# Moving the first tile's residual add and its low parts ahead of the sums in DVE's queue

## The reference

```
q_d, k_d, v_d = means over groups of 4 positions
out_d     = softmax(q_d k_d^T / 8) v_d               # 144 positions
out_up    = repeat(out_d, 4)                         # back to 576
out_local = softmax(q k^T / 8 where |i-j| < 4) v     # banded
x = out_up + out_local                               # tokens x 512
h = x @ w_in;  x = (h * tanh(softplus(h))) @ w_out   # d_ff 2048
h = x @ w_in2; s = h * softmax(h)                    # d_ff 1024
x = layernorm(s) * g_ln @ w_out2
```

## Time and profile before

| | |
|---|---|
| median of 3 runs | 734.22 us (733.68 to 735.09) |
| the profiled execution | 736.92 us, its span 735.1 us |
| PE busy | 703.1 us, 96% |
| DVE, ACT, POOL busy | 333.2, 244.1, 93.2 us |
| mean granted clock of PE | 0.981 |

### The profile page before, as it was taken

One profiled execution on the slowest core, in us unless ns is written; L12 is line 12 of the kernel. 1 busy time (PEld: TensorE's weight loads), 2 busy tenths in 40 slices (PEclk: granted clock), 3 DMA queues, 4 the chain that ended last, 5 costly groups with the idle time before them and its releaser, 6 DMA issues.

```text
span 735.1 us, 12338 instructions
## 1 busy us (share of the span) xinstructions
PE 703.1 (96%) x5152; PEld 646.4 (88%) x5152; DVE 333.2 (45%) x640; ACT 244.1 (33%) x525; POOL 93.2 (13%) x123
## 2 busy tenths in 40 slices
PE   6778779999999999999999999999999999999997
PEld 5667668999999999999999999999788888888886
DVE  7996986553222223322232332124854444445441
ACT  5676676332211211121121112115543333343432
POOL 5785760000000000000000000002000000000000
PEclk9897899999999999999999999999999999999999
DMA  8996765000000000000000000005000000000001
GB/s 227 209 264 174 224 215 217 1 1 1 1 1 0 1 1 1 1 1 0 1 1 1 1 0 1 1 1 228 1 28 17 29 15 30 15 29 15 29 15 44
DMA packets 24423, 37.50 MB, mean 51 GB/s; under 512 B 2480, under 2 KB 12720, under 8 KB 24368
## 3 DMA queue, kind: packets, MB, share of 16 engines
q1 hardware_dynamic: 24368, 36.71, 16.5%
HBM read 31.99 MB, written 4.72 MB: 50 GB/s over the span
## 4 chain that ended last, share of the span: by engine, by line
PE 81%; DVE 10%; issue 4%; ACT 3%; DMA 1%; POOL 1%; SPq 0%; POOLq 0%; DVEq 0%; ACTq 0%
PE psum L537 27%; PE psum L551 25%; PE psum L631 12%; PE psum L607 11%; PE psum L617 2%; DVE xy L930 1%; DVE xy L939 1%; DVE prob L905 1%; ACT prob L701 1%; DVE mx L902 1%; PE psum L523 1%; PE psum L508 1%; DVE wlo L1020 1%; DMA kT<-kT_dram 1%; DVE den L912 1%
## 5 line engine op out<-in xcount | busy, mean ns | idle before, releaser
L983 DVE CAST ghi<-g_sb 128x384 fp32r<-128x384 f32 x96 | 34.5, 360 | 260.9 <-PE psum L551 204.0
L725 ACT ACTIVATE g_sb<-psum 128x384 f32<-128x384 f32 x96 | 47.2, 492 | 302.8 <-PE psum L537 302.8
L537 PE MATMUL psum<-xhi,whi 128*128 128x384 f32 x384 | 129.8, 338 | 0.6 <-DVE wlo L949 0.4
L537 PE MATMUL psum<-xlo,whi 128*128 128x384 f32 x384 | 129.3, 337 | 0.0
L537 PE MATMUL psum<-xhi,wlo 128*128 128x384 f32 x384 | 129.2, 336 | 0.0
L551 PE MATMUL psum<-ghi,wlo 128*128 128x384 f32 x384 | 129.0, 336 | 0.0
L551 PE MATMUL psum<-ghi,whi 128*128 128x384 f32 x384 | 129.0, 336 | 0.0
L551 PE MATMUL psum<-glo,whi 128*128 128x384 f32 x384 | 129.0, 336 | 0.0
L537 PEld LDWEIGHTS psum<-xhi,whi 128*128 128x128 f32 x384 | 72.4, 189 | 1.4 <-ACT g_sb L725 0.7
L537 PEld LDWEIGHTS psum<-xlo,whi 128*128 128x128 f32 x384 | 72.5, 189 | 0.0
L537 PEld LDWEIGHTS psum<-xhi,wlo 128*128 128x128 f32 x384 | 72.4, 189 | 0.0
(11 more groups left out here) (95 smaller groups left out, 938.3 us busy)
## 6 DMA issues: line engine op xcount, KB each, us to landing
wraw<-w_dram SPq DMA_DIRECT2D x16, 512.0 KB, 7.1
qT<-qT_dram SPq DMA_DIRECT2D x16, 288.0 KB, 4.1
kT<-kT_dram SPq DMA_DIRECT2D x16, 288.0 KB, 6.0
v<-v_dram SPq DMA_DIRECT2D x16, 288.0 KB
out_dram<-ob SPq DMA_DIRECT2D x18, 256.0 KB, 2.0
vw<-v_dram SPq DMA_DIRECT2D x32, 128.0 KB, 4.0
wraw<-w_dram SPq DMA_DIRECT2D x4, 1024.0 KB, 7.0
vw<-v_dram SPq DMA_DIRECT2D x32, 32.0 KB, 4.0
```

The lines of the kernel that those rows point to most:

```text
L537: ins = nc.tensor.matmul(bank, a[:, w], b[:, kdx, :], start=(kdx == 0 and n == 0), stop=(kdx == KD - 1 and n == 2))
L725: nc.scalar.activation(g_sb[:, f % HR, :], psum[:, HB1 + f % HB, 0:N1], ACT.Mish).then_inc(g_ok, 1)
L983: nc.vector.tensor_copy(ghi[:, f % GR, :], g_sb[:, f % HR, :]).then_inc(ghi_ok, 1)
```

## The change

In each DVE turn the add and the low part now stand between `maxima_pooled(u)` and `sum_local(u)`, while ACT exponentiates the local scores, and no longer last in the turn. The low part of chunk 3 stays where it was, in turn 16 (it is not in the new place, since that is only reached for u < 16, and the line in turn 16 is unchanged).

```
                 if u < UNITS:
                     subtract_local(u)
                     maxima_pooled(u)
+
+                    if u in ADDED:
+                        add_pooled(0, ADDED.index(u))
+                    if u - 1 in ADDED:
+                        split_x(0, ADDED.index(u - 1))
                     sum_local(u)
...
                 if u >= LATE:
                     evict_local(u - LATE, 1)
-
-                if u in ADDED:
-                    add_pooled(0, ADDED.index(u))
-                if u - 1 in ADDED[:KD - 1]:
-                    split_x(0, ADDED.index(u - 1))
                 if u == UNITS - 1:
                     weights_in_low(0)
```

## The result

The changed kernel takes 727.7 us in the median of four runs (723.8 to 729.0), the kernel before 734.65 us; the ratio is 0.9892, 95% interval 0.9845 to 0.9939. Six more runs of it, beside 17 of the kernel before on the same chip, gave 728.2 us (726.8 to 729.4) and a ratio of 0.9911, interval 0.9887 to 0.9936. So it is faster by about 1%, 6 to 7 us. I had forecast 722.8 us, 11.4 less. By its median the first measurement lies 0.2 us beyond the upper end of my range; by its ratio, set against the 734.22 us from which I had worked, it is 726.3 us and inside. Of 11.4 us some 7 came, and what is missing needs an explanation.

A forecast was written before the change was run, and what follows sets the result against it. Attention turns: three engines nearly full, DVE most, and the add held up by POOL stops three engines. Savings 3.45 + 2.5 + 3.41 + 2.0 = 11.4 us, off the 734.2 us median: 722.8 us, range 717.0 to 727.5.

The forecast's parts named there:

- The add in its new place: Turns 3, 7, 11: the add gets POOL's pause behind pbias, takes about 0.6 us, turn 5.2 us.
- the pause on which I had set 1.7 us: Turn 7, POOL between half_qk and qd, 0.08 us long: an add missing it costs 1.7 us more.
- rival (b)'s second half: Adds of turns 7 and 11 miss POOL's pause: 2 x 1.7 us more, 726.2 us; whole rival 0.23.
- ACT's wait: ACT waited 14.4 us in four waits for the add before copying xhi; wait and following low clock would go.
- One short add stops three engines: Attention turns: a 2.52 us add left ACT idle 4.15 us and TensorE without work 4.16 us, then at 1.2 GHz.
- The low part: Turns 4, 8, 12: it waits 1.1 us for half_v and works 0.5, adding 1.5 us; turn 6.4 us.
- rival (c): Moved instructions get in between any two of POOL's; low parts cost some 0.5 us, 719.8 us; chance 0.06.
- only where POOL pauses for its own semaphore: A DVE add with two SBUF inputs gets in only at such POOL pauses, delaying POOL's next by 0.2 us.
- I keep one such pause: Turns 7 to 9: one TensorE pause costing about 5.2 us stays, so 2.5 us is saved, not 7.69.
- (a): No TensorE pause at all, instructions come in time: 16.6 us saved, 717.6 us; chance 0.20.
- (b): Losses return: second late load or instruction page, 728.0 us, or adds missing POOL's pause, 726.2; chance 0.23.
- The end: Up to the first expert product: it starts 1.4 us sooner, with 0.6 us of clock loss back, together 2.0.

The follow-up runs named there:

- adds_only: Changed kernel with only the adds moved, the low parts staying last in their turn: 725.8 us, ratio 0.9888.
- after_split: Changed kernel with the first weights' piece 0 issued in halves in SP's steps 13 and 16, piece 1 in step 17: 721.6 us, ratio 0.9833.
- after_no_v8: Changed kernel without 14 of the 16 loads of v for pooling: 720.4 us, ratio 0.9821.
- before_late: Kernel before with the two 1 MB pieces of the first weights issued in SP's steps 13 and 15, not 8 and 13: 735.0 us, ratio 1.0011.
- before_no_v8: Kernel before without 14 of the 16 loads of v for pooling: 733.9 us, ratio 0.9979.
- the early pieces: Changed kernel with both 1 MB pieces of the first weights issued in SP's steps 7 and 8: 727.55 us.

## Why the prediction was right, and where it was not

**The add in its new place** was right: 0.69, 0.69 and 0.55 us in turns 3, 7 and 11, POOL's next instruction later by 0.2 to 0.3 us, den's slack taking up most of it. In turn 7 it missed the pause on which I had set 1.7 us; it got in one instruction later, in front of kd, so that rival (b)'s second half would have been worth nothing:

```profile
43.76 0.43 POOL L402 TENSOR_TENSOR qd<-half_qk 128x144 f32<-128x144 f32 x1
...
43.91 0.69 DVE L939 TENSOR_TENSOR xy<-xy,od 128x384 f32<-128x384 f32 x1
...
44.14 0.74 POOL L402 TENSOR_TENSOR kd<-half_qk 128x144 f32<-128x144 f32 x1
```

**ACT's wait** went, and the low clock with it in turns 4 and 12 (in turns 8 and 9 the pauses kept it low, 0.77 and 0.56). As the reason of the gain it was overrated: ACT a turn later gives back 0.95 us of turns 3 and 4, the moved add 3.0 (adds_only), add and low part together 4.1. "One short add stops three engines" was true, but the engine whose stop set the length was DVE. The sum did not suffer, since I had worked it out from turns as a whole.

**The low part** was mis-sized: 1.5 us each, measured 0.72, 0.55 and 0.73 (the 0.55 in turn 8, where POOL stood waiting for v). That is rival (c), which I gave 0.06, and the rule of the Trainium skill (SBUF — State Buffer, "SBUF: two separate sides") that stands beside it: whichever instruction starts first has the ports. I had taken the place of half_v from turn 6 of the kernel before, where it began 0.03 us before pbias; behind an add POOL is later, and qd was still running. The trace of after_split, with half_v first in turn 8, has the 1.60 us, that of after_no_v8 1.46. My reading "only where POOL pauses for its own semaphore" is refuted, and the Trainium skill's rule isn't enough either: it doesn't give the 2.52 us of the old place or the 1.41 us above.

**What was left out: POOL.** I had noted that three engines are nearly full and then gave turns 5 and 6 the old 4.67 and 4.91 us. With the gaps gone, POOL has no time to catch up: turns 5, 6, 13 and 14 took 5.01, 5.44, 5.01 and 5.30 us, 1.8 us more than before in all (their sum in the kernel before is 18.98). That eats most of what the low parts saved, and adds_only shows both sides of it: with the low part in its old place turn 4 takes 6.62 us and not 5.50, but turns 5 and 6 take 4.67 and 5.10.

**The step that failed** is "I keep one such pause". First, the pause of 2.56 us was in the profiled execution of the kernel before and, as before_late and before_no_v8 suggest, mostly not in its median; I took a saving read from a span of 735.1 us off a median that lay 2.7 us below its execution. Secondly, after the change there were three in the profiled execution, and they cost 7 to 8 us: 728.2 with all loads, 720.4 without those of v. I had set down the saturation as the case against (a) and for (b), and gave (b) 0.23; its 728.0 us came nearest. The figure that I had for it was weak, though: 205 to 226 GB/s is not what a full queue moves at most, for the earlier trace rows have 282 and 306 GB/s at shares of 1.09 and 0.95, and the changed kernel moved 223 to 262 in turns 3 to 6 without a pause over 1.1 us. Without pauses on either side my terms give 3.45 + 3.36 + 3.41 + 2.0 = 12.2 us (with turns 7 to 9 of before_late, 19.63 us, in place of 23.96); 13.5 was measured.

**The end** came out near the forecast: turn 15 up to the first expert product took 6.64 us against 9.18, 2.5 saved for 2.0. The way there was another, so this is partly luck. I had let the low part of the weights decide, and half_v lose less; half_v took 1.74 us, longer than the 1.57 of before. What went is ACT's wait of 2.33 us for the add: TensorE's pooled value products of unit 13 began 4.62 us into the turn and not 7.05, and from there to the expert product it is 2.0 us in one kernel and 2.1 in the other. Behind it both kernels take the same: 735.1 - 107.35 = 627.8 and 724.8 - 97.31 = 627.5 us.

That a late page of TensorE's instructions makes the pauses is supported by their place, by the steady 2.6 to 3.0 us from packet to resumption and by the remedy, but no run took away the pages themselves, and no view shows when a page was asked for. That the transfers as a whole make them late is shown by the loads left out; how far a single load does was not settled, since the early pieces didn't lengthen the median.

## What to carry to other kernels

Take out a stall only after asking what rested in it: here the DMA queue, TensorE's instruction stream and POOL all caught up in the stalls of the add, and half of the gain went back to them. Compute the bytes per turn at the new pace and hold them against the rate and the busy share of the DMA engines in turns with the same kinds of loads (here a share near 1 went with 205 to 306 GB/s); where the engines will be full, move the loads that are not urgent in the same change. And check whether a pause in the one profiled execution is in the median of the runs before a term of the sum rests on it.

## What the runs showed of the hardware

TensorE can stop for 1 to 5 us in the middle of a row of matrix products without any semaphore, when the DMA engines are full, and the places recur from run to run (in turn 8 before the last 11 score products, in turn 9 before the last): 2.56 us in the kernel before, 3.06 and 2.19 in the changed one, 1.50 and 5.09 in its second profile. It went on 2.6 to 3.0 us behind a 16 KB packet of the queue of instructions, whatever the length of the pause. The Trainium skill (Runtime: NRT & Kernel Launch, "Instruction fetch mechanics") says that instructions are refilled in blocks of 16 KiB by a DMA queue of the sequencer, at a cost that is mostly hidden; the trace agrees in the size, and here the cost isn't hidden.

A DVE instruction with both inputs in SBUF took 0.55 us where POOL left room, 0.68 to 0.75 where it came late in a POOL instruction and got in before the next, 1.41 where one more passed it, 1.46 to 1.60 where it came shortly behind the start of one of 1.26 or 1.27 us, and 2.52 in the kernel before, where it let the rest of vd, the normalisation and one half_qk pass; the POOL instruction behind it took 0.2 to 0.3 us more. A small shift decides: begun 0.27 us ahead of half_v's record (turn 4 of the changed kernel) the low part took 0.72 us, begun 0.09 us behind it (after_split) 1.60.
